# Pair 1's gated columns kept and multiplied with the output weights in one `whole`, as pair 2's

## The chip, the cores and the metric

The kernel runs on one core of a Trainium2 chip. The metric is the device time of one execution in microseconds (us), the median of several runs. The engines of the core are called as in the profile: PE (TensorE, the matmuls), DVE (VectorE), ACT (ScalarE), POOL (GpSimd) and SP (SyncE, which here issues the DMAs; its queue serves 16 DMA engines).

## What is computed

A pooled attention gives 2304 tokens of 512 values; two feed-forward networks (FFN) follow, and they are nearly all of the work:

```python
def _moe_ref(x, w_gate, w_val, w_out, rms_g) -> np.ndarray:
    rms = np.sqrt(np.mean(x * x, axis=-1, keepdims=True) + 1e-06)
    xn = x / rms * rms_g
    g = xn @ w_gate
    silu = g * (1.0 / (1.0 + np.exp(-g)))
    val = xn @ w_val
    return (silu * val @ w_out).astype(np.float32)
...
def _moe2_ref(x, w_in, w_out) -> np.ndarray:
    h = x @ w_in
    g = h * (1.0 / (1.0 + np.exp(-h)))
    return (g @ w_out).astype(np.float32)
```

`w_gate` and `w_val` are 512 x 1536, `w_out` 1536 x 512, `w_in` 512 x 2048 and the second `w_out` 2048 x 512. The first function is FFN 1, the second FFN 2.

## The kernel before, in words

**Arithmetic.** Every number is split into a high part (type fp32r) and a low part, the rest; a product of two blocks is three matmuls, high by high, high by low, low by high. On top of this a 2 x 2 block product is made with seven block products instead of eight (Strassen-Winograd). The seven need "forms": sums and differences of blocks, of the tokens (`xt`, `xh`, `xl`), of the weights (`wt`, `wr`) and, in places, of the hidden columns.

**Phases.** The tokens are three pairs (0, 1, 2) of two blocks of 384 tokens. Six phases follow one another, as (FFN, pair): (1,0), (1,1), (2,0), (1,2), (2,1), (2,2). They are numbered 0 to 5. A phase goes through groups of 256 hidden columns, six in FFN 1, eight in FFN 2. What PE does for one matrix and one group is a *unit*: seven products of six matmuls (128 x 384), 42 in all. In FFN 1 a group has two units, G (gate) and V (value); in FFN 2 one. Units 0 to 11 are phase 0, 12 to 23 phase 1, 24 to 31 phase 2, 32 to 43 phase 3, 44 to 51 phase 4, 52 to 59 phase 5.

**Down groups, `whole` and endings.** The hidden columns of a group go to `w_out` in one of three ways. A *classic* down group (phases 0, 1 and 2) is done behind the next group's first unit (`down1` in FFN 1): the gated columns are split by ScalarE and VectorE into `ah` and `al`, PE does 48 matmuls with the group's output weights `wo`, and VectorE (`add_down`) and ScalarE add the products to `xacc`. Phase 3 (pair 2's FFN 1) is different: it keeps all gated columns in `hid`, and behind its last unit stands one *`whole`*, seven block products of 36 matmuls over all columns, 252 in all, with forms of the hidden columns (`fh`, `fl`) and folded forms of the output weights (`fw`). The last two phases end in a like way (*ending*, forms `efh`, `efl`, `ew`).

**Where the folded weights come from.** In phase 1 GpSimd makes, for each of six parts j of FFN 1's output weights, first the raw forms in `fa` (`fold_raw`: three casts and subtractions of the raw blocks themselves) and then four sums in `fb` (`fold_sums`: b0 to b5). Both are stored in DRAM (`fold_home`), from where phase 3 loads `fw` in seven loads of 1536 KB. The raw blocks come in through `raw_x` and `raw_y`.

**Memory.** Two places, `x_at[0]` and `x_at[1]`, hold the token forms of one phase each (`XHOME` says which); in phase 3 the other one holds `hid`. A ring of three slots, `wr0` to `wr2`, holds the weights of a unit. Units of the phases in which weights are made for the first time (0 and 2) get them from GpSimd and ScalarE (`weight_sums`, `weight_high`, `ring_low`) and store them in `ring_home`; the others load them back (`load_ring`), two units ahead, 1792 KB each. `wo` is stored in `out_home` in phase 0 and loaded back for phase 1 (`load_out`).

**What sets the order.** Each engine's program is written out by hand in the order of the list `items` (units, down groups, `whole`, endings). SyncE's loop goes through the same items and hangs its loads and stores on them; all of them go into one queue, which works in order of issue. `made` is the order in which GpSimd makes weights: `("r", u)` ring weights of unit u, `("o", n)` output weights of down group n, `("a", j)` and `("b", j)` the folded parts, `("c", j)` those of the endings. `keep(i)` issues the next raw block that entry `i` makes room for, waits until the entry is made, and stores it; `FOLD_AT` says behind which item. Engines wait on counting semaphores; `s_prod` counts PE's products in units, `s_wh` those in `whole`, `s_wlo` the entries GpSimd has made, `s_hd` the gated columns, `s_fhi` and `s_flo` the parts of the hidden forms. Inside a unit, ScalarE takes a snapshot of a product (`keep_first`, L1182) and VectorE adds to it (`L1561`), and PE's fourth product of the unit goes only behind that sum.

Of the kernel before, what the change touches and what calls it, by code (L numbers as in the profile page):

```python
# [20 lines left out]
def ffn_kernel(nc, q, k, v, w_gate, w_val, w_out, rms_g, w2_in, w2_out, out):  # L21
# [94 lines left out]
    classic = [ph < WHOLE for ph, _ in downs]  # L116
# [3 lines left out]
    perm0 = [PERMS * ph for ph in range(WHOLE + 1)]  # L120
# [18 lines left out]
    def split_order(n):  # L139

        if ffn_of[n] == 1:
            return GATES
        return [C22, C12, C11, C21] if ffn_of[n - 1] == 1 else [C11, C21, C22, C12]

    def lows_until(n, *blocks):
# [79 lines left out]
    C_AT = {first_unit[WHOLE + (j >= CEARLY)] + (2, 4, 6, 7, 9, 0, 1, 3)[j]: j for j in range(2 * EPART)}  # L225
# [19 lines left out]
    def raw_of(i):  # L245
# [5 lines left out]
        if kind in "ab":  # L251
            return 7 + x % 2
# [3 lines left out]
        if letter == "I":  # L256
            return (2, 0)[g] if g < 2 else 3
# [5 lines left out]
    raw_count = [sum(1 for j in range(i + 1) if raw_of(j) == raw_of(i) and made[j][0] != "b") for i in range(len(made))]  # L263
# [8 lines left out]
    o_load = {n: 16 * sum(1 for m in range(n + 1) if ("o", m) not in made_at and o_slot(m) == o_slot(n) and classic[m])  # L272
              for n in range(ND) if ("o", n) not in made_at and classic[n]}
# [11 lines left out]
    f_dram = nc.dram_tensor("fold_home", (NF, P, 2 * PART * 2 * FF), F32, kind="Internal").ap()  # L285
# [4 lines left out]
    with ctx:  # L290
# [6 lines left out]
        def sem(name):  # L297
# [13 lines left out]
        RAW = 4 * 1024  # L311


        xacc = [at(i * XACC, f"xacc{i}", [P, KC * 2 * BLOCK]) for i in range(PAIRS)]
        assert XHOME[WHOLE] == 1
# [12 lines left out]
            + [at(x_at[0] + 2 * XFORM // NF + i * RAW, f"raw_{n}", [P, 1024]) for i, n in enumerate("xy")] \  # L328
            + [at(a + 2 * RAW, f"raw_z{i}", [P, 1024]) for i, a in enumerate((0, o_at[0]))]

        hid = at(x_at[0], "hid", [P, 4, 2 * PART, BLOCK])
        part_bytes = 8 * BLOCK
        form_at = [[(ah_at, ah_at + part_bytes), (ah_at + 2 * part_bytes, ah_at + 3 * part_bytes),
                    (x_at[0] + 4 * 4 * 2 * PART * BLOCK, x_at[0] + 4 * 4 * 2 * PART * BLOCK + part_bytes)],
                   [(q_at, q_at + part_bytes), (v_at, v_at + part_bytes), (c_at, o_at[0] + 8 * PART * 2 * FF)]]
        fh = [[at(form_at[i][j][0], f"fh{i}{j}", [P, 2, BLOCK], F32R) for j in range(PART)] for i in range(2)]
        fl = [[at(form_at[i][j][1], f"fl{i}{j}", [P, 2, BLOCK], F32R) for j in range(PART)] for i in range(2)]
        fold_ring = [(last_unit[WHOLE] - 1) % RING, last_unit[WHOLE] % RING]  # L340
# [1837 lines left out]
```

## Time and profile before

| | us |
|---|---|
| median of 3 runs | 867.45 |
| lowest and highest of the 3 | 867.25, 868.26 |
| the profiled execution, a run of its own | 869.04 |
| the span of its profile | 867.3 |
| PE busy in it | 856.1 |
| VectorE busy | 551.8 |
| GpSimd busy | 428.1 |
| ScalarE busy | 354.7 |

The profiled execution took 869.04 us of which its span, from the first instruction to the last, is 867.3; 1.7 us lie outside it. Durations below come from this one execution, at the span's own clock; the medians come from the runs. All runs were at the full granted TensorE clock. A window is given in us from the start of the span. Where an engine is "busy", register, branch, semaphore and DMA-issuing instructions are not counted.

### The profile page before, as it was taken

The page shows a single profiled execution, that of the slowest core. Times are in us where ns is not written, and L with a number is a line of the kernel's source. Part 1 is how long each engine was busy: PE and PEld are TensorE (multiplying, and loading weights), DVE is VectorE, ACT ScalarE, POOL GpSimd, SP SyncE. Part 2 cuts the span into 40 slices and gives each one's busy share as a digit, 9 for nine tenths or more (in the row PEclk, how much of TensorE's full clock was granted, in tenths as well). Part 3 has the DMA queues.
Part 4 walks back from the last instruction along what each step waited for, and adds up shares of the span by engine and source line. Part 5 has one row for each costly group of instructions (what it writes and reads, how often), then busy time and mean ns, then how long its engine had stood idle before and what let it go on. Part 6 is the DMA issues. An engine that isn't in the chain of part 4 may idle for free.

```text
span 867.3 us, 13959 instructions
## 1 busy us (share of the span) xinstructions
PE 856.1 (99%) x5328; PEld 836.6 (96%) x5328; DVE 551.8 (64%) x846; ACT 354.7 (41%) x643; POOL 428.1 (49%) x433
## 2 busy tenths in 40 slices
PE   7999999999999999999999999999999999999998
PEld 6999999999999999999989899999999999999998
DVE  6689757766556767565564435569734788335873
ACT  3689745442222222445544221315433444134521
POOL 6898999883247772657864035270061700003400
PEclk9999999999999999999999999999999999999999
DMA  9971678778889995548579579997679757687762
GB/s 249 270 219 41 223 271 322 273 300 309 335 302 350 334 350 223 216 160 326 200 293 386 195 267 355 353 417 287 257 270 362 266 195 279 241 334 249 255 238 104
DMA packets 85249, 235.78 MB, mean 272 GB/s; under 512 B 22848, under 2 KB 53568, under 8 KB 73024
## 3 DMA queue, kind: packets, MB, share of 16 engines
q1 hardware_dynamic: 85184, 234.90, 75.3%
q8 instruction: 42, 0.69, 0.3%
q14 instruction: 23, 0.19, 0.1%
HBM read 159.39 MB, written 75.50 MB: 271 GB/s over the span
## 4 chain that ended last, share of the span: by engine, by line
PE 95%; DVE 2%; DMA 2%; POOL 1%; issue 0%; SPq 0%; ACT 0%; DVEq 0%; ACTq 0%; POOLq 0%
PE ps L1986 17%; PE ps L1988 16%; PE ps L1987 16%; PE ps L2121 5%; PE ps L2119 5%; PE ps L2120 5%; PE ps L2025 4%; PE ps L2027 4%; PE ps L2026 4%; PE ps L1913 3%; PE ps L2051 3%; PE ps L2052 3%; PE ps L2050 3%; PE ps L1882 2%; PE ps L2081 2%; PE ps L2080 2%
## 5 line engine op out<-in xcount | busy, mean ns | idle before, releaser
L1986 PE MATMUL ps<-xh,wr 128*128 128x384 f32 x840 | 282.5, 336 | 0.4 <-DVE qt L1561 0.4
L1988 PE MATMUL ps<-xh,wr 128*128 128x384 f32 x840 | 281.3, 335 | 0.0
L1987 PE MATMUL ps<-xl,wr 128*128 128x384 f32 x840 | 281.1, 335 | 0.0
L1986 PEld LDWEIGHTS ps<-xh,wr 128*128 128x128 f32 x840 | 157.7, 188 | 3.2 <-DVE qt L1561 1.5
L1987 PEld LDWEIGHTS ps<-xl,wr 128*128 128x128 f32 x840 | 157.8, 188 | 0.3
L1988 PEld LDWEIGHTS ps<-xh,wr 128*128 128x128 f32 x840 | 157.7, 188 | 0.0
L2119 PE MATMUL ps<-ew,efh 128*128 128x256 f32 x336 | 95.1, 283 | 0.0
L2120 PE MATMUL ps<-ew,efh 128*128 128x256 f32 x336 | 95.1, 283 | 0.0
L2121 PE MATMUL ps<-ew,efl 128*128 128x256 f32 x336 | 95.1, 283 | 0.0
L958 POOL TENSOR_TENSOR eh<-eh 128x768 f32<-128x768 f32 x8 | 17.2, 2167 | 123.4 <-DVE efl L1653 123.4
L1580 DVE TENSOR_TENSOR qt<-ps,qt 128x384 f32<-128x384 f32 x84 | 45.8, 554 | 42.2 <-PE ps L1988 42.1
L2025 PE MATMUL ps<-ah,wo 128*128 128x384 f32 x192 | 64.3, 335 | 0.8 <-DVE xacc L1611 0.8
L2121 PEld LDWEIGHTS ps<-ew,efl 128*128 128x128 f32 x336 | 64.5, 192 | 0.0
L2119 PEld LDWEIGHTS ps<-ew,efh 128*128 128x128 f32 x336 | 64.5, 192 | 0.0
L2120 PEld LDWEIGHTS ps<-ew,efh 128*128 128x128 f32 x336 | 64.5, 192 | 0.0
L2027 PE MATMUL ps<-ah,wo 128*128 128x384 f32 x192 | 64.2, 334 | 0.0
L2026 PE MATMUL ps<-al,wo 128*128 128x384 f32 x192 | 64.2, 334 | 0.0
L1653 DVE TENSOR_TENSOR efl<-eh,efh 128x768 fp32r<-128x768 f32 x56 | 59.8, 1123 | 5.1 <-ACT efh L1277 5.1
L938 POOL TENSOR_TENSOR ebt<-raw_z 128x256 f32<-128x256 f32 x8 | 5.9, 738 | 110.6 <-PE ps L2081 39.9
L1277 ACT ACTIVATE efh<-eh 128x768 fp32r<-128x768 f32 x56 | 43.0, 834 | 41.2 <-PE ps L2121 41.2
L1198 ACT ACTIVATE qt<-qt 128x384 f32<-128x384 f32 x78 | 39.9, 523 | 39.9 <-DVE qt L1580 39.5
L1569 DVE TENSOR_TENSOR qt<-ps,qt 128x384 f32<-128x384 f32 x42 | 23.4, 557 | 50.2 <-PE ps L1988 50.2
(198 smaller groups left out, 1744.9 us busy)
## 6 DMA issues: line engine op xcount, KB each, us to landing
wr<-ring_home SPq DMA_DIRECT2D x40, 1792.0 KB, 9.2
ring_home<-wr SPq DMA_DIRECT2D x20, 1792.0 KB, 8.1
ew<-ending_home SPq DMA_DIRECT2D x8, 2048.0 KB, 8.1
out_home<-wo SPq DMA_DIRECT2D x14, 1024.0 KB, 9.3
ew<-out_home SPq DMA_DIRECT2D x24, 512.0 KB, 6.9
fw<-fold_home SPq DMA_DIRECT2D x7, 1536.0 KB, 7.9
ending_home<-eb SPq DMA_DIRECT2D x16, 512.0 KB, 10.4
raw_c<-in_moe_w_out SPq DMA_DIRECT2D x13, 512.0 KB, 7.5
```

Of the source, the lines that this page charges most:

```text
L1277: act.activation(efh[e][i % 2][:, 2 * j:2 * j + 2, :], ending_part(f, j), ACT.Copy).then_inc(s_ehi, 1)
L1580: dve.tensor_tensor(done if units[u][1] == "V" else qt[:, c, :], done, tiles(u)[:, c, :], ALU.add)\
L1653: dve.tensor_tensor(efl[e][i % 2][:, 2 * j:2 * j + 2, :], ending_part(f, j), efh[e][i % 2][:, 2 * j:2 * j + 2, :], ALU.subtract).then_inc( ...
L1986: pe.matmul(out_ps, w_hi, x_hi, start=first and c == 0, stop=False, skip_group_check=True)
L1987: pe.matmul(out_ps, w_hi, x_lo, start=False, stop=False, skip_group_check=True)
L1988: ins = pe.matmul(out_ps, w_lo, x_hi, start=False, stop=c == 1, skip_group_check=True)
L2025: pe.matmul(out_ps, w_hi, h_hi, start=(rot or ends[0]) and c == 0, stop=False, skip_group_check=True)
L2026: pe.matmul(out_ps, w_hi, h_lo, start=False, stop=False, skip_group_check=True)
L2027: ins = pe.matmul(out_ps, w_lo, h_hi, start=False, stop=(rot or ends[1]) and c == 1, skip_group_check=True)
L2119: pe.matmul(out_ps, h_hi, w_hi, start=first and c == 0, stop=False, skip_group_check=True)
L2120: pe.matmul(out_ps, h_hi, w_lo, start=False, stop=False, skip_group_check=True)
L2121: ins = pe.matmul(out_ps, h_lo, w_hi, start=False, stop=c == 2 * EPART - 1, skip_group_check=True)
```

## The change

Phase 1 becomes a phase of the second kind. `WHOLES` is now (1, 3): phase 1 has no down groups, its gated columns stay in a `hid0` of its own, and one `whole` of 252 matmuls stands behind unit 23. For this `XHOME` changes, so that `x_at[0]` is free in phase 1 for the hidden columns, and the token forms of later phases change places.

GpSimd makes only the sums, b0 to b5. Their buffer is doubled (`fb0`, `fb1`), each stored with two DMAs of 512 KB, and the third sum waits for the store of the first. The raw forms are no longer made: `load_fold` takes them in three pieces from `out_home`, where the output weights of phase 0 are already kept in high and low parts. The six reloads of `wo` go.

Much shares memory with these buffers: `fb1` and the `raw_x`, `raw_y` blocks lie in `hid0`, `fh` lies in part in the same place. So ScalarE's first copies to `fh` and VectorE's gates of phase 1's last groups wait for the last sum's store, and ring weights for units 24 to 26 are made around and during the `whole`, when a ring slot comes free (`fold_free`). The new raw buffer `raw_h` lies in `hid0` too.

```diff
-    WHOLE, ENDINGS = 3, (4, 5)
-
-    XHOME = [0, 1, 0, 1, 1, 1]
+    WHOLES, ENDINGS = (1, 3), (4, 5)
+
+    XHOME = [0, 1, 1, 0, 0, 0]
...
-            pending = None if ph >= WHOLE else len(downs)
+            pending = None if ph in WHOLES + ENDINGS else len(downs)
             downs.append((ph, g))
-        if ph == WHOLE:
+        if ph in WHOLES:
             items.append(("whole", ph))
...
-    for j in range(2 * PART):
-        made += [("a", j), ("b", j)]
-    FOLD_AT = {}
-    for i, entry in enumerate(made[-4 * PART:]):
-        g, u = i // 3, 2 * GROUPS[1] + 2 * (i // 3) + 1
-        FOLD_AT[(("down", GROUPS[1] - 1 + g), ("unit", u), ("unit", u + 1))[i % 3]] = entry
+    made += [("b", j) for j in range(2 * PART)]
+    FOLD_AT = {("unit", first_unit[1] + 1 + j): ("b", j) for j in range(2 * PART)}
+    f_pieces = [PART if fw < 3 else 1 for _, fw, _, _ in WPRODUCTS]
+    f_load = [[16 * sum(f_pieces[m] * (e + (m <= i)) for m in range(i % 3, NF, 3)) for i in range(NF)] for e in range(2)]
     U2, N2 = first_unit[2], last_down[1] + 1
+
...
+    fold_free = {U2 + 1: 2 * 5, U2 + 2: 2 * 6}
     made += [("r", U2), ("r", U2 + 1), ("o", N2)]
...
+        hid_at = [x_at[1 - XHOME[ph]] for ph in WHOLES]
+        hid = [at(a, f"hid{e}", [P, 4, 2 * PART, BLOCK]) for e, a in enumerate(hid_at)]
...
-        fa = at(x_at[0] + 5 * XFORM // NF, "fa", [P, 3, 2, FF], F32R)
-        fb = at(o_at[1], "fb", [P, 4, 2, FF], F32R)
...
+        fb_at = (o_at[1], x_at[0] + HID - RAW // 2)
+        fb = [at(a, f"fb{i}", [P, 4, 2, FF], F32R) for i, a in enumerate(fb_at)]
...
+                elif made[i] == ("r", U2 + 1):
+
+                    sp.wait_ge(s_flo, PART * 4)
...
-                if made[i] == ("r", U2 + 1):
-                    sp.wait_ge(s_bst, 16 * 2 * PART)
+                if made[i] in (("r", U2 + 2), ("o", N2)):
+                    sp.wait_ge(s_wh, 2 * (NF - 1))
...
-                if kind in "ab":
-                    lo, hi = (0, 3) if kind == "a" else (3, NF)
-                    sp.dma_start(f_dram[lo:hi, :, 2 * FF * x:2 * FF * (x + 1)].rearrange("f p n -> p f n"),
-                                 fold_bits[kind]).then_inc(s_ast if kind == "a" else s_bst, 16)
+                if kind == "b":
+                    for a in range(2):
+                        sp.dma_start(f_dram.rearrange("f p (g a c n) -> p f g a c n", a=2, c=2, n=FF)[:, :, x // 2, a, x % 2, :],
+                                     fb_bits[x % 2][:, :, a, :]).then_inc(s_bst[x % 2], 16)
...
+                if f < 3:
+
+                    g, cols = PART if f else 0, slice(FF * (f == 2), FF * (f == 2) + FF)
+                    for j in range(PART):
+                        sp.dma_start(home[:, j, :, :],
+                                     o_dram[g + j, :, :].rearrange("p (b n) -> p b n", n=DM)[:, :, cols])\
+                          .then_inc(s_fw[i % 3], 16)
+                else:
+                    sp.dma_start(home.rearrange("p g b n -> p (g b n)"), f_dram[f - 3, :, :]).then_inc(s_fw[i % 3], 16)
...
-                if item == ("unit", first_unit[1]):
-                    load_raw(made_at["a", 0])
-                    load_raw(made_at["a", 1])
-                if item == ("unit", last_unit[1] - 2):
-                    load_raw(made_at["r", U2 + 1])
...
+                if item == ("unit", last_unit[0]):
+                    load_raw(made_at["b", 0])
+                    load_raw(made_at["b", 1])
...
+                        if item == ("whole", WHOLES[0]) and i == 5:
+                            load_raw(made_at["r", U2 + 1])
+                if item == ("whole", WHOLES[0]):
+                    load_raw(made_at["o", N2])
+                    load_raw(made_at["r", U2 + 2])
...
-                if kind == "down":
-                    for n in range(x + 1, ND):
-                        if classic[n] and o_before(n) == x and ("o", n) not in made_at:
-                            load_out(n)
...
+                if u in fold_free:
+                    pool.wait_ge(s_wh, fold_free[u])
...
+                pool.wait_ge(s_raw[raw_of(i)], 16 * raw_count[i])
+                if j >= 2:
+                    pool.wait_ge(s_bst[j % 2], 32 * (j // 2))
...
-                pool.tensor_copy(fa[:, 0:2, 0, :], r[:, :, 0:FF])
-                pool.tensor_copy(fa[:, 2, 0, :], r[:, 1, FF:2 * FF]).then_inc(s_fold, 1)
-                pool.wait_ge(s_fold, 2 * j + 1)
-                pool.tensor_tensor(fa[:, 0:2, 1, :], r[:, :, 0:FF], fa[:, 0:2, 0, :], ALU.subtract)
-                pool.tensor_tensor(fa[:, 2, 1, :], r[:, 1, FF:2 * FF], fa[:, 2, 0, :], ALU.subtract).then_inc(s_wlo, 1)
...
+                if made[i] == ("r", U2):
+                    whole_sums(0)
...
+                        act.wait_ge(s_hd, hd0[n + j + 1])
+                        act.wait_ge(s_down, down0[n])
+                        if e == 0:
+                            act.wait_ge(s_bst[1], 32 * PART)
...
+                    if e == 0 and i >= 5:
+                        weight_high(made_at["r", U2 + 1], ((0, 1), (2,))[i - 5])
...
-                if x == U2 - 1:
-                    weight_high(made_at["r", U2 + 1])
+                if x in (U2 - 2, U2 - 1):
+                    weight_high(made_at["r", U2], ((0, 1), (2,))[x - U2 + 2])
...
-                if ph == WHOLE and (letter, g) == ("G", PART):
-                    form_high(0)
...
+                if ph in WHOLES and (letter, g) == ("G", (PART + 1, PART)[WHOLES.index(ph)]):
+                    form_high(WHOLES.index(ph), 0)
...
+                if downs[n][0] == WHOLES[0] and downs[n][1] > PART:
+                    dve.wait_ge(s_wlo, made_at["b", 2 * PART - 1] + 1)
+                    dve.wait_ge(s_bst[1], 32 * PART)
...
-                if ph == WHOLE and 2 * PART + 1 <= x - first_unit[ph] <= 3 * PART:
-                    form_low(0, [x - first_unit[ph] - 2 * PART - 1])
+                if ph in WHOLES:
+                    e = WHOLES.index(ph)
+                    form_low(e, 0, ({9: (0,), 10: (1, 2)}, {7: (0,), 8: (1,), 9: (2,)})[e].get(x - first_unit[ph], ()))
...
-            def whole(ph):
+            def whole(e):
+                ph = WHOLES[e]
                 for i, (bank, _, _, first) in enumerate(WPRODUCTS):
-                    pe.wait_ge(s_fw[i % 3], 16 * (i // 3 + 1))
+                    pe.wait_ge(s_fw[i % 3], f_load[e][i])
```

How this stands in the engines' programs: first SyncE, the issues behind the end of units 13 to 16 in phase 1. `wr` are ring slots, `raw_x` and `raw_y` the raw blocks of output weights, `fa`, `fb` the forms that are stored, `wo0` the reloaded output weights. Before:

```order
L629 DMA wr1<-ring_home 128x3584 [waits ring_stored1,product_made]
L581 DMA raw_x<-in_moe_w_out 128x2x512 [waits w_lo_made]
L606 DMA fold_home<-fb 128x4x512 [waits w_lo_made]
L629 DMA wr2<-ring_home 128x3584 [waits ring_stored2,product_made]
L606 DMA fold_home<-fa 128x3x512 [waits w_lo_made]
L677 DMA wo0<-out_home 128x2048 [waits out_w_stored0,down_made]
L581 DMA raw_y<-in_moe_w_out 128x2x512 [waits w_lo_made]
L606 DMA fold_home<-fb 128x4x512 [waits w_lo_made]
L629 DMA wr0<-ring_home 128x3584 [waits ring_stored0,product_made]
```

After:

```order
L630 DMA wr1<-ring_home 128x3584 [waits ring_stored1,product_made]
L583 DMA raw_x<-in_moe_w_out 128x2x512 [waits w_lo_made]
L607 DMA fold_home<-fb0 128x4x256 [waits w_lo_made]
L607 DMA fold_home<-fb0 128x4x256
L630 DMA wr2<-ring_home 128x3584 [waits ring_stored2,product_made]
L583 DMA raw_y<-in_moe_w_out 128x2x512 [waits w_lo_made]
L607 DMA fold_home<-fb1 128x4x256 [waits w_lo_made]
L607 DMA fold_home<-fb1 128x4x256
L630 DMA wr0<-ring_home 128x3584 [waits ring_stored0,product_made]
```

The stores of `fa` and the reloads of `wo0` are gone, each store of sums is two halves from alternating buffers, and one comes with every unit instead of every second.

Second, ScalarE around unit 20 (phase 1). `qt` and `vt` are snapshots and Silu results of a unit, `ah` the high parts of gated columns for a classic down group, `fh000` to `fh002` the three parts of the first hidden form. Before, units 20 to 22:

```order
L1182 ACTIVATE qt<-ps 128x384 [waits gated,product_made]
L1215 ACTIVATE ah<-vt 128x384 [waits down_made,gated] x3
L1195 ACTIVATE qt<-ps 128x384 [waits gated,product_made]
L1198 ACTIVATE qt<-qt 128x384 [waits combined] x3
L1182 ACTIVATE vt<-ps 128x384 [waits hidden_lo_made,product_made]
L1215 ACTIVATE ah<-vt 128x384 [waits down_made,gated]
L1182 ACTIVATE qt<-ps 128x384 [waits gated,product_made]
```

After, unit 20 to the beginning of unit 22:

```order
L1175 ACTIVATE qt<-ps 128x384 [waits gated,product_made]
L1188 ACTIVATE qt<-ps 128x384 [waits gated,product_made]
L1191 ACTIVATE qt<-qt 128x384 [waits combined]
L1245 ACTIVATE fh000<-hid0 128x768 [waits fold_sums_stored1,down_made,gated]
L1245 ACTIVATE fh001<-hid0 128x768 [waits fold_sums_stored1,down_made,gated]
L1245 ACTIVATE fh002<-hid0 128x768 [waits fold_sums_stored1,down_made,gated]
L1191 ACTIVATE qt<-qt 128x384 [waits combined] x2
L1175 ACTIVATE vt<-ps 128x384 [waits combined,product_made]
L1175 ACTIVATE qt<-ps 128x384 [waits gated,product_made]
```

The `ah` copies are gone. Three `fh` copies stand behind unit 20's first Silu, with a wait for the stores of `fb1`; two Silus and unit 21's snapshot (`vt`) stand behind them.

## Rows read from the trace of the kernel before

**Rows 1.** The page: busy us by engine; DMA tenths and GB/s by slice.

```profile
PE 856.1 (99%) x5328; PEld 836.6 (96%) x5328; DVE 551.8 (64%) x846; ACT 354.7 (41%) x643; POOL 428.1 (49%) x433
...
DMA  9971678778889995548579579997679757687762
GB/s 249 270 219 41 223 271 322 273 300 309 335 302 350 334 350 223 216 160 326 200 293 386 195 267 355 353 417 287 257 270 362 266 195 279 241 334 249 255 238 104
```

**Rows 2.** Waits of PE: what it waited for, us in total, times, longest.

```profile
PE ps L2025 <- DVE xacc L1611: 0.8, 1, 0.8
```

**Rows 3.** Windows: us; busy PE, PEld, DVE, ACT, POOL; clock; DMA share; GB/s.

```profile
239.00:377.59 138.59, 137.79 (x793) 137.35 (x793) 92.74 (x144) 40.77 (x80) 81.68 (x85) 1.00 0.80 293
501.81:582.92 81.11, 80.92 (x463) 80.05 (x462) 44.29 (x79) 18.70 (x38) 41.48 (x40) 1.00 0.96 353
582.92:626.60 43.68, 43.68 (x253) 43.68 (x253) 38.03 (x48) 21.12 (x29) 2.42 (x2) 1.00 0.75 287
```

**Rows 4.** Windows: phase 1's second down group and its fourth.

```profile
276.49:284.81 8.32, 8.32 (x49) 8.32 (x49) 7.11 (x11) 2.46 (x4) 8.02 (x8) 1.00 0.97 387
322.35:331.74 9.39, 8.60 (x49) 8.28 (x49) 7.50 (x11) 3.31 (x5) 4.67 (x4) 1.00 0.97 391
```

**Rows 5.** Timeline of GpSimd, one fold sum: start, us, line, operation.

```profile
239.19 0.74 POOL L916 TENSOR_TENSOR fbt<-raw_x 128x256 f32<-128x256 f32 x1
...
244.56 1.29 POOL L926 TENSOR_TENSOR fb<-fbt,fb 128x512 fp32r<-128x512 f32 x1
```

**Rows 6.** Timeline of GpSimd, ring weights of unit 25.

```profile
354.17 0.74 POOL L866 TENSOR_TENSOR wt<-raw_a 128x256 f32<-128x256 f32 x1
354.87 1.46 POOL L867 TENSOR_TENSOR wt<-raw_a 128x256 f32<-128x256 f32 x1
...
360.99 1.31 POOL L888 TENSOR_TENSOR wr<-wt,wr 128x512 fp32r<-128x512 f32 x1
```

**Rows 7.** Timeline of PE and ScalarE, units 38 and 39 (pair 2).

```profile
538.42 0.33 PE L1986 MATMUL ps<-xh,wr 128*128 128x384 f32 x1
...
544.62 2.30 ACT L1247 ACTIVATE fh<-hid 128x768 fp32r<-128x768 f32 x3
...
547.66 0.47 ACT L1182 ACTIVATE vt<-ps 128x384 f32<-128x384 f32 x1
...
548.87 0.45 PE L1986 MATMUL ps<-xh,wr 128*128 128x384 f32 x1
```

**Rows 8.** Timeline of SyncE: start and duration of issues.

```profile
223.94 1.56 SPq L581 DMA_DIRECT2D raw_x<-in_moe_w_out  x1
...
246.50 0.32 SPq L629 DMA_DIRECT2D wr<-ring_home  x1
...
554.53 0.91 SPq L610 DMA_DIRECT2D ending_home<-eb  x2
560.65 0.33 SPq L629 DMA_DIRECT2D wr<-ring_home  x1
```

**Rows 9.** DMA view, issues at 531.2, 554.9, 560.6: KB, us to landing.

```profile
wr<-ring_home SPq DMA_DIRECT2D x1, 1792.0 KB, 7.0
...
ending_home<-eb SPq DMA_DIRECT2D x1, 512.0 KB, 11.9
...
wr<-ring_home SPq DMA_DIRECT2D x1, 1792.0 KB, 10.4
```

**Rows 10.** Windows, columns as in rows 3: four stretches.

```profile
8.00:25.00 17.00, 12.98 (x96) 11.52 (x96) 11.49 (x18) 7.80 (x15) 12.13 (x14) 1.00 1.18 266
254.00:271.00 17.00, 17.00 (x100) 17.00 (x99) 8.38 (x17) 2.56 (x6) 9.33 (x11) 1.00 0.88 331
246.50:302.00 55.50, 55.50 (x321) 55.48 (x320) 39.41 (x61) 14.53 (x30) 34.79 (x37) 1.00 0.93 341
520.00:585.00 65.00, 64.81 (x371) 64.03 (x370) 38.02 (x67) 13.45 (x28) 34.28 (x32) 1.00 1.00 374
```

**Rows 11.** GpSimd's groups by form, 510 to 600: busy us, mean ns, idle before.

```profile
L971 POOL TENSOR_TENSOR hid<-hid 128x768 f32<-128x768 f32 x3 | 5.5, 1847 | 0.0
```

More of the change, by code:

```diff
@@ L119, in ffn_kernel @@
     lo0 = [4 * sum(classic[:n]) for n in range(ND + 1)]
-    perm0 = [PERMS * ph for ph in range(WHOLE + 1)]
+    perm0 = [PERMS * sum(1 for i in range(ph) if i not in WHOLES + ENDINGS) for ph in range(len(PHASES))]
     hd0 = [4 * sum(1 for f in ffn_of[:n] if f == 1) for n in range(ND + 1)]
@@ L224, in ffn_kernel @@
     CEARLY = 5
-    C_AT = {first_unit[WHOLE + (j >= CEARLY)] + (2, 4, 6, 7, 9, 0, 1, 3)[j]: j for j in range(2 * EPART)}
+    C_AT = {first_unit[ENDINGS[0] if j >= CEARLY else WHOLES[1]] + (2, 4, 6, 7, 9, 0, 1, 3)[j]: j for j in range(2 * EPART)}
     c_before = [max((m for m in range(j) if CHOME[m] == CHOME[j]), default=None) for j in range(2 * EPART)]
@@ L262, in ffn_kernel @@
                 for i in range(len(made))]
-    raw_count = [sum(1 for j in range(i + 1) if raw_of(j) == raw_of(i) and made[j][0] != "b") for i in range(len(made))]
+    raw_count = [sum(1 for j in range(i + 1) if raw_of(j) == raw_of(i)) for i in range(len(made))]
     sums0 = [3 * sum(1 for m in made[:i] if m[0] in "rbc") for i in range(len(made) + 1)]
@@ new lines, in ffn_kernel @@
+        fold_ring = [[(last_unit[ph] - 1) % RING, last_unit[ph] % RING] for ph in WHOLES]
+        fw = [[at(a, f"fw{e}{i}", [P, PART, 2, 2, FF], F32R) for i, a in
+               enumerate((o_at[0], ring_at[fold_ring[e][0]], ring_at[fold_ring[e][1]]))] for e in range(2)]
+        fb_at = (o_at[1], x_at[0] + HID - RAW // 2)
+        assert fb_at[1] + 2 * RAW == x_at[0] + 2 * XFORM and raw[8] is not None
+        fb = [at(a, f"fb{i}", [P, 4, 2, FF], F32R) for i, a in enumerate(fb_at)]
+        fbt = [at(a, f"fbt{i}", [P, 4, 2, FF]) for i, a in enumerate(fb_at)]
@@ L504, in ffn_kernel @@
         s_ost = [sem(f"out_w_stored{i}") for i in range(2)]
-        s_oload = [sem(f"out_w_loaded{i}") for i in range(2)]
         s_xt, s_xhi, s_xlo = sem("x_sum_made"), sem("x_hi_made"), sem("x_lo_made")
@@ L1048, in _, with whole_sums @@
             ring_low(made_at["r", 1], (2,))
+            def whole_sums(e):
+                for f in (3, 5):
+                    for j in range(PART):
+                        hidden_sums(e, f, j)
             for i in range(2, MADE):
@@ L1361, in act_unit @@
                         silu(x, i)
-                if ph == WHOLE and (letter, g) == ("G", PART):
-                    form_high(0)
+                        if classic[n] and before["unit", x] and before["unit", x][0] == "whole":
+                            high(n, i)
+                if ph in WHOLES and (letter, g) == ("G", (PART + 1, PART)[WHOLES.index(ph)]):
+                    form_high(WHOLES.index(ph), 0)
                 if ph in ENDINGS and g - EPART in (1, 2):
@@ L1437, in _ @@
                     weight_high(made_at["r", 2 * g + 2])
-                if ph < 5:
-                    for f in HIGH_AT["late" if ph == 1 else PHASES[ph][0]].get(g, ()):
+                if classic[n]:
+                    for f in HIGH_AT[PHASES[ph][0]].get(g, ()):
                         token_high(ph + 1, f)
-                if x == N2 - 2:
-                    weight_high(made_at["r", U2])
                 if letter == "I" and classic[n]:
@@ L1767, in dve_unit @@
                 combine_last(x, C21)
+                if classic[n] and before["unit", x] and before["unit", x][0] == "whole":
+                    low(n, 0)
                 if letter == "V":
@@ L2150, in _ @@
                 elif kind == "whole":
[L2151 removed]
+                    whole(WHOLES.index(x))
                 elif kind == "ending":
```

357 lines of the change are left out of this document (165 added, 192 removed).

## The prediction

> **What bounds the kernel.** I read the page first: TensorE (PE) is busy 856.1 of 867.3 us [rows 1]. Then the waits of PE: the longest inside an FFN is 0.8 us for VectorE's `xacc` [rows 2]. So what counts is how many matmuls PE issues, and whether a new wait stops it. Everything else matters only where it makes PE late. The other resource near its limit is the DMA engines: the 12th to the 15th of its 40 slices (238 to 325 us, this stage) carry the digits 8 and 9 [rows 1].
>
> **What PE no longer does.** One stretch of the kernel before, 239.00 to 377.59, holds what the change rewrites: units 13 to 24 and the six down groups of pair 1's FFN 1, 138.59 us. The later FFN 1 (pair 2) already has the new form: its last eleven units took 81.11 us (462 matmuls; the row counts one of a neighbour), its `whole` 43.68 us [rows 3]. With one more unit at 7.32 us (below), the same work is 81.11 + 43.68 + 7.32 = 132.11 us if pair 1 copies that: **6.5 us less**. Checked by counting: a down group is 48 matmuls in 8.32 us, six are 288; a `whole` is 252, so 36 matmuls of 0.173 us go, 6.2 us. The fourth down group was 1.07 us longer than its fellows (9.39 against 8.32) [rows 4], by the `xacc` wait of [rows 2], and goes as well; against that, bare units with no down group between them lose 0.8 us to small stops: 81.11 against eleven times 7.30, where 7.30 is (138.59 - 5 x 8.32 - 9.39) / 12. So 6.2 + 1.07 - 0.8 = 6.5. These terms need no cover: they are on PE.
>
> **What is moved beside PE, and costs nothing if its cover holds.** GpSimd's raw forms (`fa`, two casts and two subtractions, six times) and their six stores go; the six reloads of `wo` go; the sums (`fb`) stay, at 6.7 us each undisturbed [rows 5]. VectorE loses its 24 `add_down` and the low parts of six groups, ScalarE their high parts; both idle beside PE. The weights of the first three units of the next phase are now made during `whole`: the slot of unit 25 comes free after product 4, 12.5 us before `whole` ends, and unit 25 starts 7.3 us behind that end; one unit's weights took GpSimd 8.1 us from the first sum to the last subtraction, ScalarE's copies between them included (354.17 to 362.30) [rows 6], and fit in 19.8 us. Pair 2's stages keep their order; three of its seven `fw` loads become three pieces each, with two products (12.5 us) to land in.
>
> **The new wait.** ScalarE's first three copies to `fh` now wait until the last store of odd fold sums (b5) has landed. They stand in unit 20, and behind them in ScalarE's order are two Silus and the snapshot with which unit 21 begins; PE cannot start unit 21's fourth product before that snapshot and VectorE's sum of it. The deadline, from pair 2's twin of this place: unit 38 started at 538.42, its `fh` copies at 544.62, 6.2 us later, unit 39's snapshot at 547.66, and PE's fourth product came at 548.87, 0.11 us late [rows 7]. So the copies may start 6.2 us behind the start of their unit, and every us more is a us of PE. Units last 7.32 us ((538.42 - 501.81) / 5, the first time from [rows 7], the second the edge of a stretch of [rows 3]); in the new kernel unit 13 still starts at 239.00, unit 20 at 290.25, and the deadline is **296.45**. VectorE's gates of unit 21 wait for the same store, but stand behind that snapshot's sum, later in the unit, so they add nothing unless the store is later still.
>
> **When does that store land?** Order of the queue from 246.50, where unit 13 ends [rows 8]: ring load, raw block, store of b0; ring load, raw block, store of b1; and so on. b0 and b1 are ready by then: the first raw block is issued at 223.94 before, behind a ring load [rows 8], and both now stand ahead of that load. Up to and with b5's store the queue holds six ring loads, four raw blocks and twelve half stores: 6 x 1.835 + 4 x 0.524 + 12 x 0.524 = 19.4 MB (a ring load is 1792 KB, the others 512 KB each [rows 9]). What moves in a full queue: 374 GB/s in the 65 us of pair 2's same stage, at a DMA share of 1.00 [rows 10]. In an empty queue a ring load lands 7.0 us after its issue; in a full one, 560.65 + 10.4 = 571.1 against the store before it, the second of the two issued in the 0.91 us from 554.53, so 555.0 + 11.9 = 566.9, it takes 4.2 us [rows 8, 9]. So the start costs up to 2.8 us over the rate; I take half, 1.35. The last store lands at 246.5 + 1.35 + 19.4 / 0.374 = **299.7**.
> Does GpSimd, not the queue, decide? With that rate the stores of b0 to b3 land at 257.0, 266.1, 275.2 and 284.3 (3.41 MB, 9.1 us a round). A sum of 7.3 us (6.7 plus some disturbance) starts when the store two before it has landed, so b5 is ready at 291.6 and its store issued at 292 to 293, while ring load 21 is in the queue until 296.9. The queue decides, by 4 us. Ring loads 20, 21 and 22 land at 289.2, 296.9 and 304.6, each just ahead of its unit.
> The stop is 299.7 - 296.45 = **3.3 us**. A stop of that length costs no clock: between 8 and 25 us PE was busy 12.98 of 17 us at a granted clock of 1.00, the 2.4 GHz level [rows 10]. **Sum:** -6.5 + 3.3 = -3.2 us. The profiled execution took 869.04 us (span 867.3, 1.7 outside it) and the median of the runs is 867.45; the difference is applied to the median: 864.3. On the profiled run it would be 865.8.
>
> [rows 10] show 374 GB/s at share 1.00, and 417 in the page's best slice [rows 1]. The Trainium skill, page DMA: Bandwidth & Descriptors, section Where 436 GB/s comes from, gives a ceiling of 435 GB/s for the DMA fabric and about 358 GB/s for what one core draws from HBM. The trace goes above the second for 65 us on end, so 358 is not a limit here; an estimate by it would be a landing at 302 and a time of 866.6; one by 435 would be a landing at 292 and no stop at all, my first rival below.
>
> **Rivals.**
> *No stop.* If the queue moves 399 GB/s or more over 49 us, the store lands by 296.45: 867.45 - 6.5 = 861.0. For it: the best slices reach 417. Against it: they are mostly reads; here a third of the bytes are stores in rows of 1 KB, and the stretch with such stores at share 1.00 gave 374.
> *The queue falls behind (slower than before).* Place: the same store. Price: at the 331 GB/s of 254 to 271, a stretch of the old stage with the old stores [rows 10], 19.4 / 0.331 = 58.6 us, landing at 306.5, a stop of 10.1 us, ring loads 20 to 22 late inside it: 871.1. It decides from 341 GB/s (landing 304.7, 0.2% slower); even is at 353. For it: 246.5 to 302 of the old kernel gave 341. Against it: at a share of 0.93, so with gaps the new, fuller queue would not have; 341 / 0.93 is 367.
> *A second wait at the entry of `whole`.* GpSimd makes unit 24's ring weights only after unit 21's products, waits for a ScalarE copy that stands in unit 23, and only then makes the hidden sums of product 1 (1.85 us each [rows 11]). Counted from unit 22's start: the copy stands behind the first snapshots of unit 23 (from 7.3) and ends at about 10, two subtractions of 1.3 [rows 6] end the weights at 12.6, three sums of 1.85 end at 18.1, and product 1 asks behind two units and one product, at 14.6 + 6.24 = 20.9. Cover 2.8 us. Where VectorE disturbs it, a GpSimd operation of 0.74 us takes up to 1.46 [rows 6]; if the cover is gone, about 3 us: 867.3.
> *The change does not remove work.* Excluded: PE's stream has 36 matmul rows fewer.
>
> **Chances.** Forecast (a rate of 353 to 399) 0.56, time 864.3, its own range 861.5 to 867.5; no stop 0.20; falls behind 0.14; second wait 0.10. A measurement tells about 0.2%, 1.7 us, from no change. Faster by more: no stop 0.20, the part of the forecast above 364 GB/s 0.42, together 0.62. Same: 0.12 of the forecast, 0.09 of the second wait, 0.02 of the queue case: 0.23. Slower: 0.12 of the queue case and the rest, 0.15. The range reaches from no stop (861.0) to 869.5, a landing at 305, and leaves most of the slow case out.
>
> **What would show it.** Right: a stop of PE of 2 to 5 us at about 300 us of the span, in unit 21, its waits ending with ScalarE's snapshot and before that ScalarE idle until `fold_home<-fb` lands; GpSimd's last fold sum done at about 292, before the queue is; a DMA share near 1.00 and some 374 GB/s between 246 and 300; a `whole` of 43.7 us twice; no wait of PE between that `whole` and unit 26. Wrong: PE running through unit 21 (then the rate was higher), a stop of PE at a product whose weights are late (then the ring loads, not the snapshot, are last), GpSimd busy with b5 at 297 or later, or a stop inside the first `whole` with `hid` or `fl` as its releaser.

## The result

| | us |
|---|---|
| changed kernel, median of 10 runs | 870.19 (868.44 to 871.44) |
| kernel before, median of 10 runs, the three above among them | 868.06 (867.25 to 869.57) |
| changed over before | 1.0024, 95% interval 1.0014 to 1.0033 |
| profiled execution of the changed kernel, and its span | 869.81, 868.1 |

The change makes the kernel slower, by 0.14 to 0.33%. Forecast were 864.3 us and a range of 861.0 to 869.5; the time lies above it. The most likely case was faster. All medians in this text are of fast executions: one of early_both's seven (1042.45 us) and one of the nine of the kernel before that ran beside spread (3004.75 us) were slow and are left out.

### The profile page after: what moved, and what is told of

The parts are those of the page before. It is cut to its first block, busy times and chain, and to the rows that moved or that the text cites. A ratio compares the mean times of both kernels' runs of the same rounds, so it can differ in the third digit from the quotient of the medians.

```text
span 868.1 us, 13900 instructions
## 1 busy us (share of the span) xinstructions
PE 852.5 (98%) x5292; PEld 831.6 (96%) x5292; DVE 554.8 (64%) x835; ACT 359.5 (41%) x640; POOL 423.6 (49%) x415
## 4 chain that ended last, share of the span: by engine, by line
PE 61%; DVE 1%; issue 1%; ACT 0%; DVEq 0%
PE ps L1993 10%; PE ps L1995 10%; PE ps L1994 10%; PE ps L2131 5%; PE ps L2130 5%; PE ps L2129 5%; PE ps L2089 3%; PE ps L2090 3%; PE ps L2091 3%; PE ps L2060 3%; PE ps L2061 3%; PE ps L2059 3%; DVE hid L1632 0%; DVE fl L1625 0%; ACT fh L1245 0%
## 5 line engine op out<-in xcount | busy, mean ns | idle before, releaser
L1993 PE MATMUL ps<-xh,wr 128*128 128x384 f32 x840 | 283.6, 338 | 3.2 <-DVE vt L1564 2.9
L1993 PEld LDWEIGHTS ps<-xh,wr 128*128 128x128 f32 x840 | 158.2, 188 | 7.1 <-DVE vt L1564 3.3
L1175 ACT ACTIVATE qt<-ps 128x384 f32<-128x384 f32 x42 | 20.7, 492 | 105.0 <-PE ps L1995 104.6
L2089 PE MATMUL ps<-fh,fw 128*128 128x384 f32 x168 | 56.4, 336 | 2.7 <-DVE fl L1625 1.8
L2091 PE MATMUL ps<-fh,fw 128*128 128x384 f32 x168 | 56.2, 334 | 0.0
L2090 PE MATMUL ps<-fl,fw 128*128 128x384 f32 x168 | 56.2, 334 | 0.0
```

The costliest lines, as they stand in the source:

```text
L1993: pe.matmul(out_ps, w_hi, x_hi, start=first and c == 0, stop=False, skip_group_check=True)
L2089: pe.matmul(out_ps, w_hi, h_hi, start=first and c == 0, stop=False, skip_group_check=True)
L2090: pe.matmul(out_ps, w_hi, h_lo, start=False, stop=False, skip_group_check=True)
L2091: ins = pe.matmul(out_ps, w_lo, h_hi, start=False, stop=c == 2 * PART - 1, skip_group_check=True)
```

## The profile after

The page's first two parts, which answer to [rows 1], with the row of PE's clock:

```profile
PE 852.5 (98%) x5292; PEld 831.6 (96%) x5292; DVE 554.8 (64%) x835; ACT 359.5 (41%) x640; POOL 423.6 (49%) x415
...
PEclk9999999999999999999999999999999999999999
DMA  9971678778869967567579579997779757687762
```

The 36 matmuls are gone (5328 to 5292), and PE is 3.6 us less busy. But the span grew by 0.8 us (867.3 to 868.1), so PE stands still for longer. PE's clock row shows nothing of what follows: a slice is 21.7 us, and 3 us at half clock in it still round to a 9. The waits of PE, whose longest inside an FFN was 0.8 us [rows 2], name the places (line, what it waited for, us in total, times, longest):

```profile
PE ps L1993 <- DVE vt L1564: 2.9, 1, 2.9
PE ps L2089 <- DVE fl L1625: 1.8, 2, 1.1
...
PE ps L2089 <- issue: 0.9, 1, 0.9
```

L1993 is a matmul of a unit, L2089 the first of three in `whole`. Windows of the changed kernel, columns as in [rows 3]: units 13 to 23, the queue's full stretch, the stop in unit 21, the stretch behind it, the first `whole` and the second.

```profile
238.61:323.65 85.04, 82.19 (x463) 81.44 (x463) 45.06 (x79) 20.15 (x41) 40.88 (x42) 0.98 0.83 317
246.09:299.00 52.91, 52.91 (x305) 52.63 (x305) 28.69 (x51) 9.98 (x21) 26.33 (x28) 1.00 1.01 387
300.16:303.35 3.19, 0.34 (x2) 0.02 (x1) 0.56 (x1) 2.45 (x5) 0.00 (x0) 0.94 1.00 418
303.35:306.40 3.05, 3.05 (x10) 3.05 (x10) 0.69 (x2) 0.00 (x0) 0.00 (x0) 0.50 0.98 391
323.65:370.86 47.21, 44.49 (x254) 43.59 (x254) 45.94 (x47) 22.89 (x32) 23.31 (x13) 1.00 0.64 227
583.70:627.38 43.68, 43.68 (x253) 43.68 (x253) 38.03 (x48) 21.11 (x29) 3.11 (x2) 1.00 0.80 295
```

Three things are to be seen: the stop, the half clock behind it, and a longer `whole`. Units 13 to 23 took 85.04 us where pair 2's eleven took 81.11 [rows 3]: 3.0 us of stop in the third row, and behind it a row at a granted clock of 0.50, the 1.2 GHz level, in which the matmuls stood 0.32 us apart instead of 0.17, some 1.4 us lost in all (these eleven units took 4.4 us more than in spread, below, which has no stop). And the first `whole` took 47.21 us where the second, of the same 252 matmuls, took 43.68: 3.5 us.

The first stop is the predicted one. The timeline of ScalarE and the queue's issues before it (start, duration; last, in brackets, the idle time before and what ended it):

```profile
290.70 0.91 SPq L607 DMA_DIRECT2D fold_home<-fb  x2
...
295.69 0.52 ACT L1191 ACTIVATE qt<-qt 128x384 f32<-128x384 f32 x1
299.10 2.31 ACT L1245 ACTIVATE fh<-hid 128x768 fp32r<-128x768 f32 x3 [2.89 <-DMA fold_home<-fb]
301.32 0.92 ACT L1191 ACTIVATE qt<-qt 128x384 f32<-128x384 f32 x2
302.14 0.47 ACT L1175 ACTIVATE vt<-ps 128x384 f32<-128x384 f32 x1
```

ScalarE stood 2.89 us in front of the `fh` copies, until b5's last store had landed at 299.00; two Silus and the snapshot came behind them, and PE, due at 300.3, went on at 303.35. In the prediction's own terms: unit 20 started at 289.90, so the copies might begin at 296.1 (6.2 us later); they began 3.0 us after that.

The stops inside `whole` are another matter. GpSimd's and VectorE's timelines at its entry, changed kernel:

```profile
319.05 1.29 POOL L890 TENSOR_TENSOR wr<-wt,wr 128x512 fp32r<-128x512 f32 x1 [3.99 <-ACT wr L1119]
320.30 1.29 POOL L891 TENSOR_TENSOR wr<-wt,wr 128x512 fp32r<-128x512 f32 x1
321.54 5.77 POOL L964 TENSOR_TENSOR hid<-hid 128x768 f32<-128x768 f32 x3
327.28 7.57 POOL L968 TENSOR_TENSOR hid<-hid 128x768 f32<-128x768 f32 x3
...
326.52 6.64 DVE L1625 TENSOR_TENSOR fl<-hid,fh 128x768 fp32r<-128x768 f32 x3 [0.92 <-ACT fh L1245]
333.09 4.32 DVE L1632 TENSOR_TENSOR hid<-hid 128x768 f32<-128x768 f32 x3
337.33 2.68 DVE L1625 TENSOR_TENSOR fl<-hid,fh 128x768 fp32r<-128x768 f32 x3
...
341.68 2.68 DVE L1625 TENSOR_TENSOR fl<-hid,fh 128x768 fp32r<-128x768 f32 x3
344.28 0.95 DVE L1534 TENSOR_TENSOR xt<-xacc,xt 128x768 f32<-128x768 f32 x1
345.15 0.54 DVE L1649 TENSOR_TENSOR xacc<-ps,xacc 128x384 f32<-128x384 f32 x1
```

and the same lines before, at the entry of pair 2's `whole`:

```profile
574.42 5.46 POOL L971 TENSOR_TENSOR hid<-hid 128x768 f32<-128x768 f32 x3
579.83 3.66 POOL L975 TENSOR_TENSOR hid<-hid 128x768 f32<-128x768 f32 x2
585.05 1.84 POOL L975 TENSOR_TENSOR hid<-hid 128x768 f32<-128x768 f32 x1 [1.55 <-DVE hid L1591]
...
585.82 3.63 DVE L1618 TENSOR_TENSOR fl<-hid,fh 128x768 fp32r<-128x768 f32 x3 [0.91 <-ACT fh L1247]
589.37 2.68 DVE L1625 TENSOR_TENSOR hid<-hid 128x768 f32<-128x768 f32 x3
```

In pair 2 GpSimd has nearly ended its six hidden sums when VectorE begins its low parts. In pair 1 it begins them when unit 24's weights are made, 5 us before VectorE begins its low parts, and the two work side by side: VectorE's three low parts take 6.6 us instead of 3.6, its sums 4.3 instead of 2.7. PE stopped inside product 1 and in front of products 2 and 3, at 331.8, 337.3 and 344.6, by 1.25, 0.92 and 1.05 us. The first two stops ended with a low part of VectorE. The profile names no releaser for the third ("issue"), but PE's program waits there for VectorE's sum L1649, which ended at 345.69; PE went on at 345.79:

```profile
345.79 0.41 PE L2089 MATMUL ps<-fh,fw 128*128 128x384 f32 x1 [0.89 <-issue]
```

That sum stood behind the late low parts in VectorE's order, so all three stops are VectorE's lateness.

## The experiments

Theories, as they stood. A: the stop in unit 21 is the store of b5, through ScalarE's order. D: the stops in `whole` are the contention of GpSimd and VectorE. Rivals: B, the queue as a whole stops PE; E, VectorE's own list at the entry of `whole` is too long. The table compares on each profile one stretch, from the start of unit 13 to the start of the last ending's last matmul, since unit 13 starts at 237.5 to 239.6 us in these profiles. Each ratio is taken against runs of the kernel before from the same session: their medians were 868.06 for the changed kernel, 868.07 for the four kernels below it in the table, 867.62 for more_store, tiny_early and all_three, and 867.20 for spread. So compare kernels of different sessions by the ratio or the stretch.

| kernel | median us | over before (95%) | stretch us | units 13 to 23 | first `whole` |
|---|---|---|---|---|---|
| before | 867.20 to 868.07 | 1 | 625.15 | | |
| changed | 870.19 | 1.0024 (1.0014 to 1.0033) | 626.31 | 85.04 | 47.21 |
| part2_late | 865.67 | 0.9974 (0.9964 to 0.9983) | 622.29 | 80.63 | 47.19 |
| stores_early | 865.25 | 0.9972 (0.9960 to 0.9984) | 621.93 | 80.73 | 47.20 |
| copy_early | 868.34 | 1.0002 (0.9987 to 1.0016) | 625.30 | 87.28 | 43.68 |
| early_both | 864.80 | 0.9964 (0.9953 to 0.9976) | 622.36 | 84.34 | 43.69 |
| more_store | 871.76 | 1.0050 (1.0035 to 1.0065) | 628.58 | 87.09 | 47.23 |
| tiny_early | 861.99 | 0.9934 (0.9920 to 0.9949) | 618.64 | 80.69 | 43.68 |
| all_three | 862.96 | 0.9948 (0.9931 to 0.9964) | 619.94 | 80.87 | 44.70 |
| spread | 862.46 | 0.9941 (0.9927 to 0.9955) | 618.83 | 80.68 | 43.68 |

### The copies moved out of the snapshot's way: part2_late

```diff
-                        if e == 0:
+                        if e == 0 and j == 2:
                             act.wait_ge(s_bst[1], 32 * PART)
...
-                    form_high(WHOLES.index(ph), 0)
+                    form_high(WHOLES.index(ph), 0, range(3 if ph == WHOLES[1] else 2))
+                if x == U2 - 3:
+                    form_high(0, 0, (2,))
```

> Only ScalarE's order changes: the third part of the first hidden form (the only one that shares memory with the second sum buffer) is copied behind unit 21's snapshot, and only it waits for the last sum's store. Theory A (the store at 299 us stops PE because a snapshot is queued behind the copies): the 3.0 us stop in unit 21 is gone, the store still lands at about 299, and the 1.4 us at half clock behind the stop are gone too; 870.2 - 4.4 = 865.8, the three stops inside the first whole (3.5 us) stay. Rival B (ring loads or something else of the queue stop PE at the same place): the stop moves to weights of unit 22 or to VectorE's gates and the time stays within 1 us of 870.2.

Measured 865.67. The timeline of ScalarE in it:

```profile
296.72 1.57 ACT L1245 ACTIVATE fh<-hid 128x768 fp32r<-128x768 f32 x2
298.19 0.95 ACT L1191 ACTIVATE qt<-qt 128x384 f32<-128x384 f32 x2
299.07 0.49 ACT L1175 ACTIVATE vt<-ps 128x384 f32<-128x384 f32 x1
299.79 0.85 ACT L1245 ACTIVATE fh<-hid 128x768 fp32r<-128x768 f32 x1 [0.23 <-DMA fold_home<-fb]
```

The store landed at 299.68, as late behind unit 13's start as before (60.5 and 60.4 us). Only nothing stood behind it any more. The stop and the half clock are gone, `whole` is unchanged. A holds, B falls.

### The stores one unit earlier: stores_early

```diff
-    FOLD_AT = {("unit", first_unit[1] + 1 + j): ("b", j) for j in range(2 * PART)}
+    FOLD_AT = {("unit", first_unit[1] + j): ("b", j) for j in range(2 * PART)}
```

> Each store of sums is issued one unit earlier (b0 behind unit 12 instead of 13), into the stretch 240 to 246 us in which the queue was empty. Theory A: the queue and the chain of buffers shift by about 7 us, the last store lands at about 292, before the deadline of 296; no stop in unit 21, 865.8. Rival (the queue's total is the bound and the shift gains only the empty 6 us at the full rate): it lands at 293 to 296, still no stop. Rival C (bytes after 299 are late instead): ring load of unit 22 or 23 stops PE, 867 or more.

Measured 865.25; b5's last store landed at 289.8, 52.0 us behind unit 13's start, 8.4 us earlier, and so earlier than either expectation had it. There is no stop in units 21 to 23. Another edit of the same cause has the same effect, and rival C falls. That is the test of A from the other side: there the waiting was moved, here the landing.

### One more store: more_store

```diff
+                    if x == 5:
+                        sp.dma_start(spare.rearrange("f p (u n) -> p f u n", n=FF)[:, :, 0, :],
+                                     fb_bits[1][:, :, 0, :]).then_inc(s_bst[1], 16)
...
-                            act.wait_ge(s_bst[1], 32 * PART)
+                            act.wait_ge(s_bst[1], 32 * PART + 16)
...
-                    dve.wait_ge(s_bst[1], 32 * PART)
+                    dve.wait_ge(s_bst[1], 32 * PART + 16)
```

> The changed kernel with one more 512 KB store of half of b5 to a spare place, which the same waits include. Theory A (PE waits for the queue to finish b5's stores): the last store lands 1.35 us later, at 300.4, the stop of unit 21 grows from 3.0 to about 4.4 us; 870.2 + 1.4 = 871.6, plus what ring loads 22 and 23, also 1.35 us later, may add. Rival (the copies were held by something else): unchanged at 870.2. The stretch at half clock behind the stop stays at some 10 matmuls if its length does not depend on the stop, and grows by a third if it does.

Measured 871.76. PE's wait, and two windows: the last part of the stop and the stretch behind it:

```profile
PE ps L1997 <- DVE vt L1568: 4.1, 1, 4.1
```

```profile
303.49:305.60 2.11, 0.00 (x1) 0.00 (x1) 0.56 (x1) 1.36 (x4) 0.00 (x0) 0.50 1.02 435
305.60:310.25 4.65, 4.65 (x15) 4.65 (x16) 1.46 (x3) 0.00 (x0) 0.00 (x0) 0.50 1.01 376
```

The extra store landed at 301.24, 61.7 us behind unit 13's start, where the changed kernel's last store landed 60.4 us behind it: 1.27 us later. The stop grew from 3.02 to 4.29 us over the usual spacing, by the same 1.27; 512 KB at 387 GB/s would be 1.35 us. So what the store takes in the queue comes out of PE one to one. The stretch at half clock behind the stop grew from ten matmuls to fifteen, by half and not by the third that was expected, and the clock had fallen while PE still stood. The time hit the expected 871.6 partly by luck: by the ratios, and by the stretches, this kernel is 2.3 us above the changed one, of which 1.3 are the stop and 0.8 the clock; the session's own runs of the kernel before were 0.4 us faster.

### GpSimd's weights ended earlier: copy_early and early_both

```diff
-                if x in (U2 - 2, U2 - 1):
-                    weight_high(made_at["r", U2], ((0, 1), (2,))[x - U2 + 2])
+                if x == U2 - 2:
+                    weight_high(made_at["r", U2])
```

Early_both has the edit of stores_early as well.

> ScalarE's copy of unit 24's weight sums is moved from unit 23 to unit 22 (ScalarE was idle there from 311.6 to 314.4), so GpSimd ends these weights at about 317.6 instead of 321.6 and starts the hidden sums 4 us earlier. Theory D (the three stops inside the first whole, 3.5 us, come from GpSimd's hidden sums running beside VectorE's low parts and sums, each slowing the other): stops shrink to about 1 us, 870.2 - 2.5 = 867.7; the stop in unit 21 stays at 3.0. Rival E (VectorE's own list is too long at the entry of whole, whatever GpSimd does): no change, 870.2.

> Both edits, stores one unit earlier and the weight copy in unit 22. If A and D hold and do not depend on one another: 870.2 - 4.4 - 2.5 = 863.3, faster than the kernel before by 0.5%. If unit 21's earlier end only makes the entry of whole tighter (the fold weights or ring loads late): 865 or more.

Measured 868.34 and 864.80, where 867.7 and 863.3 were expected. Copy_early is 1.85 us faster than the changed kernel. Early_both is 0.45 us faster than stores_early by the medians and 0.4 us slower by the stretches, so the runs tell no difference. `whole` did what D expected, and more: 43.68 and 43.69 us, no stop left. That already speaks against E. But a stop of 1.95 us stood in unit 23 now, and behind it in early_both 3.2 us at half clock. Timelines of GpSimd and VectorE in early_both, and two windows behind the stop:

```profile
313.12 6.85 POOL L964 TENSOR_TENSOR hid<-hid 128x768 f32<-128x768 f32 x3
...
312.61 3.88 DVE L1625 TENSOR_TENSOR fl<-hid,fh 128x768 fp32r<-128x768 f32 x2
316.40 0.55 DVE L1564 TENSOR_TENSOR vt<-ps,vt 128x384 f32<-128x384 f32 x1
```

```profile
317.00:318.53 1.53, 1.52 (x9) 1.53 (x9) 0.16 (x1) 0.00 (x0) 1.53 (x2) 1.00 0.96 225
318.53:321.71 3.18, 3.18 (x12) 3.18 (x11) 1.51 (x3) 0.00 (x0) 3.18 (x2) 0.50 0.96 410
```

The contention had only moved: GpSimd's sums, 4 us earlier, now ran beside VectorE's two low parts at the end of unit 22, which took 3.9 us instead of 1.8, and the sum that PE waits for stood behind them. The expectation had the first half of this right and had missed the second.

### The contention taken away: tiny_early

```diff
+                if e == 0:
+                    b11, b12, b22 = b11[:, :, 0:8], b12[:, :, 0:8], b22[:, :, 0:8]
```

It has the edit of stores_early as well. It leaves out most of GpSimd's sums, so it does not compute the result; it only shows what their time is worth.

> Stores one unit earlier, and GpSimd's six hidden sums for the first whole are made over 8 of 384 tokens only (the rest of these sums is left out, VectorE's and PE's work stays). Theory D (contention between GpSimd and VectorE makes the stops inside whole): VectorE's three low parts at the entry of whole take 3.6 instead of 6.6 us, its sums 2.7 instead of 4.3, whole is 43.7 us instead of 47.2: 865.25 - 3.5 = 861.7. Rival E (VectorE's list is too long by itself): whole stays above 46 us, 865.

Measured 861.99. VectorE's timeline at the entry of `whole`:

```profile
322.04 2.69 DVE L1627 TENSOR_TENSOR fl<-hid,fh 128x768 fp32r<-128x768 f32 x3 [0.91 <-ACT fh L1247]
324.65 2.69 DVE L1634 TENSOR_TENSOR hid<-hid 128x768 f32<-128x768 f32 x3
```

With VectorE's list untouched, the low parts took 2.7 us instead of 6.6 and `whole` 43.68. D holds, E falls. Stores_early is the pair to compare with: 865.25 to 861.99, 3.3 us, where the profiles' stretches differ by 3.29.

### A version without the contention: all_three and spread

Both have the edits of early_both; shown is what comes on top.

```diff
+                if x == U2 - 2:
+                    form_low(0, 0, (1,))
...
-                    form_low(e, 0, ({9: (0,), 10: (1, 2)}, {7: (0,), 8: (1,), 9: (2,)})[e].get(x - first_unit[ph], ()))
+                    form_low(e, 0, ({9: (0,), 10: (2,)}, {7: (0,), 8: (1,), 9: (2,)})[e].get(x - first_unit[ph], ()))
```

> The two edits of the run before (stores one unit earlier, weight copy in unit 22), and VectorE's low parts of the first hidden form spread: part 0 at the end of unit 21, part 1 in the middle of unit 22, part 2 at its end. Theory F (the 1.95 us stop of unit 23 in the two runs with the early copy comes from two low parts at the end of unit 22 running beside GpSimd's hidden sums, ahead of the sum that PE waits for): the stop and the 1.5 us at half clock behind it go, whole stays at 43.7; 865.2 - 3.4 = 861.8. Rival G (one low part beside GpSimd, or one in mid-unit, is enough to be late): a stop of 0.5 to 1.5 us in unit 22 or 23, 863 to 864.5.

Measured 862.96, between the two expectations: the stop of unit 23 is down to 0.15 us, but the last hidden sums still ran beside VectorE's first low parts in `whole` (5.0 us for three), and two stops of 0.55 and 0.25 us are left there. So in spread the low parts moved once more (part 1 stands at the end of unit 21), and GpSimd's first hidden sum went into time in which it was idle. Against all_three:

```diff
+                if x == U2 - 3:
+                    form_low(0, 0, (0,))
...
-                    form_low(0, 0, (1,))
+                    form_low(0, 0, (2,))
...
-                    form_low(e, 0, ({9: (0,), 10: (2,)}, {7: (0,), 8: (1,), 9: (2,)})[e].get(x - first_unit[ph], ()))
+                    form_low(e, 0, ({9: (1,)}, {7: (0,), 8: (1,), 9: (2,)})[e].get(x - first_unit[ph], ()))
...
+                if made[i] == ("r", U2):
+                    hidden_sums(0, 3, 0)
```

> The kernel with three edits, its low parts moved once more: part 0 to unit 21 behind the first sum (VectorE idle there for 1.4 us), part 1 at the end of unit 21, part 2 in the middle of unit 22, so that none is beside GpSimd's hidden sums; and GpSimd makes the first of these sums ahead of unit 24's weights, in time in which it was idle. Theory F: no stop is left in units 22, 23 and whole, whole 43.7 us, and the time equals that of the kernel with tiny sums, 862.0. Rival G: GpSimd's first sum makes VectorE late in unit 21, or unit 24's weights later in unit 22: a new stop there, 863 or more.

Measured 862.46, ratio 0.9941. Two windows, units 13 to 23 and the first `whole`:

```profile
239.05:319.73 80.68, 80.68 (x463) 80.07 (x463) 44.77 (x79) 20.16 (x41) 47.18 (x44) 1.00 0.89 330
319.73:363.41 43.68, 43.68 (x253) 43.68 (x253) 41.74 (x47) 22.89 (x32) 15.81 (x11) 1.00 0.68 253
```

PE is busy to the last hundredth in both. The stretch is 618.83 us, with all the work done, against 618.64 for tiny sums and 625.15 before. This version computes the whole result and is faster than both kernels, by 0.6% than the one before; its ratio and all_three's are too close for the runs to tell them apart.

## Why the prediction failed, step by step

- **PE's work, -6.5 us: right.** With nothing in the way the stretch is 6.3 us shorter (spread). Units without down groups took 80.7 us for eleven, where 81.11 was taken.
- **The store's landing at 299.7: right, in part by luck.** 299.00, at 387 GB/s where 374 was taken from [rows 10], with a share of 1.01. With 19.4 MB that rate would give 297.6. But 52.91 us at 387 GB/s are 20.5 MB: 1.1 MB moved that the sum did not count. The only other transfers of the program then issued stood behind b5's stores (ring loads at 291.7 and 297.4, `fw` loads from 297.9), so later transfers ran beside earlier ones. The two errors nearly cancel. (Half of 2.8 is 1.4, not the 1.35 of the sum; that is nothing here.) Counted from unit 13, which began 0.4 us earlier, 60.4 us against 60.7. The queue, not GpSimd, decided as forecast: b5 was made at 290.7 and the ring load ahead of it in the queue landed only at 296.3. The rivals on this rate (no stop, queue behind) are out.
- **The stop of 3.3 us: right,** 3.0.
- **"A stop of that length costs no clock": wrong,** 1.4 us in the profile. The row brought for it, 8 to 25 us in [rows 10], has 4 us of idle time, but in pieces; the longest single wait of PE in it is 1.3 us. The row did not bear the sentence.
- **No stop in `whole`: wrong,** 3.5 us. The second-wait rival had the place and GpSimd's times to a few tenths. From unit 22's start at 309.00: copy ended 10.0 (forecast 10), weights 12.6 (12.6), three sums 18.3 (18.1). The cover of 2.8 us was there. What failed is that only GpSimd's chain was laid against PE's demand. VectorE's work in the same us was not priced, though [rows 6] shows an operation of 0.74 us taking 1.46 beside it. VectorE took 3.0 us longer for three low parts, against a cover that was counted on GpSimd's side. The prediction's own sign of being wrong, a stop inside the first `whole` with `fl` as its releaser, is what came.

In sum: -6.5 + 3.0 + 1.4 + 3.5 = +1.4 us, the forecast of PE's work with the measured prices of the rest, and 626.31 - 625.15 = +1.2 measured on the profiles. The medians differ by 2.1, and the interval of the ratio reaches from 1.2 to 2.9 us. Nine of the ten runs had a mean granted clock under 1 (0.996 to 0.998), and the one at 1.000 was the fastest, at 868.44: the clock's part is in nearly all runs, and not of one size. That one run lies 0.4 us above the median before, and the sum without the clock's 1.4 is 0.0. How much of the 0.9 us between medians and profiles is that stays open.

The chances failed too. The first mistake was to treat the second wait as an alternative to the stop. They lie some 30 us apart (300.2 and 331.8) and both came. Added up, 864.3 + 3 + 1.4 = 868.7, and 0.6 us more because the kernel before came out at 868.06 in ten runs and not at 867.45: 869.3, against 870.19.

## What to carry to other kernels

When work moves to an idle engine or to another time, lay out what VectorE does in the same microseconds as GpSimd, not each against PE alone: two engines that slow one another have no cover, however much idle time each has. Before a wait for a transfer is put into an engine's order, look at what stands behind it there; taking it to the other side of a snapshot was worth 4 us here, as much as getting the transfer 8 us earlier. And a row that shows many short gaps proves nothing about one long gap.

## What the runs showed of the hardware

- **GpSimd and VectorE.** A low part (two inputs in SBUF, 128x768) takes VectorE 0.9 us alone, and a GpSimd sum 1.85. At the entry of the changed kernel's first `whole`, three of each side by side (in ns: shortest, median, longest) took:

```profile
L1625 DVE TENSOR_TENSOR fl<-hid,fh x3: 1607/2592/2593, 326.5 to 330.6; 128x768 fp32r<-128x768 f32 x3
L968 POOL TENSOR_TENSOR hid<-hid x3: 2542/2552/2554, 327.3 to 332.3; 128x768 f32<-128x768 f32 x3
```

  The Trainium skill, page SBUF — State Buffer, section SBUF: two separate sides, says that such a VectorE instruction and a GpSimd one hold a port pair in turn, each for its whole length, so that the loser waits. Waiting for each other's whole length would be, as an estimate, 0.9 + 1.85 = 2.75 us for each. The trace agrees in kind and nearly in size: 2.59 and 2.55 where both engines had one operation after another.
- **The clock of TensorE.** Behind stops of 3.0 and 4.3 us (changed, more_store) and of 2.0 us in unit 23 (early_both) PE ran at a granted clock of 0.50, the 1.2 GHz level, for 3.05, 4.65 and 3.18 us. In more_store the clock had fallen 2.1 us before PE went on; in early_both it was still 1.00 for the first 1.5 us behind the stop; behind the stops of 1.25 us and less in `whole` it stayed 1.00. In copy_early's profile the same 1.95 us stop of unit 23 was not followed by such a stretch (the first stop, of 3.0 us, was), and of that kernel's ten runs the two at a mean clock of 1.000 took 866.6 and 866.7 us, the others, at 0.994 to 0.998, 867.7 to 871.1. Of early_both's six, three at 1.000 took 863.3 to 864.4 us and three at 0.998 took 865.2 to 865.8. So the same program pays the clock for its stops in some executions and not in others (a mean clock of 0.998 or less in nine of ten of the changed kernel, eight of ten of copy_early, three of six of early_both). It is a reason to take such a stop out even where its own length seems affordable.
- **The DMA queue.** 387 GB/s for 53 us at a share of 1.01; 6.3 of its 20.5 MB were stores in rows of 1 KB. The forecast had taken 374 and counted such stores against a higher rate; the stretch was no slower for them than the 374 to 391 GB/s of [rows 4] and [rows 10] at a share near 1.
